# Attention scores of the three upper block levels, limited to the queries and keys that are read

## What is computed

```python
f = 1.0 / (1.0 + np.exp(-f_logit))
state = np.zeros((B, H, D, D), dtype=np.float32)
for t in range(S):
    state = f[:, :, t, :, None] * state + np.einsum('bhd,bhe->bhde', k[:, :, t], v[:, :, t])
    y[:, :, t] = np.einsum('bhd,bhde->bhe', q[:, :, t], state)
```

## Time and profile before

| | |
|---|---|
| median of 3 runs | 1319.17 us (1318.1 to 1324.99) |
| profiled execution, its own time | 1315.64 us |
| its span, first to last instruction | 1314.0 us |
| TensorE, matmuls | 1246.3 us busy, 95% |
| TensorE, stationary loads | 1148.2 us busy, 87% |
| VectorE | 859.2 us busy, 65% |
| ScalarE | 458.8 us busy, 35% |
| GpSimd | 454.3 us busy, 35% |

### The profile page before, as it was taken

One profiled execution on the slowest core, in us unless ns is written; L12 is line 12 of the kernel. 1 busy time (PEld: TensorE's weight loads), 2 busy tenths in 40 slices (PEclk: granted clock), 3 DMA queues, 4 the chain that ended last, 5 costly groups with the idle time before them and its releaser, 6 DMA issues.

```text
span 1314.0 us, 26515 instructions
## 1 busy us (share of the span) xinstructions
PE 1246.3 (95%) x8915; PEld 1148.2 (87%) x8916; DVE 859.2 (65%) x1939; ACT 458.8 (35%) x982; POOL 454.3 (35%) x376
## 2 busy tenths in 40 slices
PE   4899999999899999999999999599999999999998
PEld 3787887877798999989999898499999999999997
DVE  6888898885477878778787787344444544444433
ACT  3565566554222232222322222332332323233221
POOL 8558787654623506060536440310010101010000
PEclk9999999999999999999999999799999999999999
DMA  6233333253613131313313510210010101010000
GB/s 213 66 105 119 125 115 120 82 178 107 228 69 139 41 144 36 144 48 132 144 36 120 184 44 25 78 37 28 28 54 1 55 18 38 18 36 18 0 18 18
DMA packets 36175, 105.46 MB, mean 80 GB/s; under 512 B 4992, under 2 KB 20352, under 8 KB 33664
## 3 DMA queue, kind: packets, MB, share of 16 engines
q1 hardware_dynamic: 27504, 56.41, 13.0%
q0 software_dynamic: 8592, 47.98, 10.3%
HBM read 77.83 MB, written 26.54 MB: 79 GB/s over the span
## 4 chain that ended last, share of the span: by engine, by line
PE 76%; POOL 9%; DVE 7%; ACT 4%; issue 4%; DMA 1%; DVEq 0%; POOLq 0%; ACTq 0%
PE pD L1750 12%; PE pD L1859 10%; PE pA L1859 10%; PE pS L1782 8%; PE pA L1782 8%; PE pA L1873 7%; PE pA L1559 5%; PE pA L1750 4%; PE pS L1873 3%; PE pA L1764 2%; POOL fT L563 1%; PE pX L1724 1%; POOL prods L598 1%; DVE W L1070 1%; POOL we L688 1%
## 5 line engine op out<-in xcount | busy, mean ns | idle before, releaser
L1496 DVE TENSOR_TENSOR gs<-pD,sig 128x384 f32<-128x384 f32 x96 | 53.5, 557 | 199.6 <-ACT sig L1005 199.6
L1246 DVE STREAM_TRANSPOSE pA<-pD 32x128 f32<-32x128 f32 x416 | 138.3, 332 | 54.5 <-PE pD L1750 48.7
L739 POOL DMA_INDIRECT pair<-y_sorted,y_row x48 | 46.5, 969 | 340.7 <-DVE z L1475 271.7
L1246 DVE STREAM_TRANSPOSE pA<-pA 32x128 f32<-32x128 f32 x400 | 133.0, 332 | 44.0 <-PE pA L1750 38.4
L1559 PE MATMUL pA<-W 64*128 64x128 f32 x1920 | 141.6, 289 | 16.3 <-DVE W L1070 12.2
L909 ACT ACTIVATE hidH<-pA 128x512 fp32r<-128x512 f32 x110 | 65.5, 599 | 250.0 <-DVE pA L1246 246.4
L1559 PEld LDWEIGHTS pA<-W 64*128 64x128 f32 x1920 | 119.9, 192 | 34.8 <-DVE W L1070 18.7
L1750 PE MATMUL pD<-we,xsH 128*128 x462 | 146.0, 397 | 2.8 <-issue 2.8
L1782 PE MATMUL pA<-we,hidH 128*128 (+1 forms) x464 | 120.7, 341 | 0.0
L1005 ACT ACTIVATE sig<-pD 128x384 f32<-128x384 f32 x96 | 47.2, 491 | 210.4 <-PE pA L1859 210.4
L1070 DVE TENSOR_TENSOR W<-W,prods 128x512 f32<-128x512 f32 (+1 forms) x120 | 98.8, 829 | 28.9 <-PE pA L1559 26.8
(11 more groups left out here) (260 smaller groups left out, 2887.1 us busy)
## 6 DMA issues: line engine op xcount, KB each, us to landing
stage<-w POOLq DMA_DIRECT2D x14, 1536.0 KB, 8.9
qk<-qk_t SPq DMA_DIRECT2D x24, 512.0 KB, 3.7
xs<-x_sorted SPq DMA_DIRECT2D x55, 192.0 KB, 2.4
y_sorted<-yo SPq DMA_DIRECT2D x55, 192.0 KB, 1.9
fT<-f_t SPq DMA_DIRECT2D x12, 512.0 KB, 4.3
vN<-v_n SPq DMA_DIRECT2D x24, 256.0 KB, 2.7
out<-fin SPq DMA_DIRECT2D x8, 576.0 KB, 2.8
stage<-w SPq DMA_DIRECT2D x2, 1536.0 KB, 9.5
```

The source lines that it names most:

```text
L739: pool.indirect_dma_start(out=pair[:, j, k], out_offset=None, in_=y_sorted[:, :], in_offset=bass.IndirectOffsetOnAxis(ap=y_row[:, t * TS + ...
L1246: ins = dve.transpose(by_32[1][32 * q:32 * (q + 1), :, i], by_32[0][32 * i:32 * (i + 1), :, q])
L1496: dve.tensor_tensor(gs[:], pD[:, f % 2 * 512:f % 2 * 512 + TT], sig[f % 2][:], ALU.mult).then_inc(s_u, 1)
```

## The change

From level 3 on, `scores` hands the matmul fewer columns: of the keys (stationary) those up to the end of the last first half, 128 - h, and of the queries (moving) only the second halves', 64 of 128. The output shrinks in the same way: 128 - h partitions, and in each group of 128 columns only the second halves' columns, which are written where they were before. Level 3 has h = 16 (112 keys, queries in runs of 16), level 4 h = 32 (96 keys, runs of 32), level 5 h = 64 (64 keys, one run of 64). The number of matmuls, their order, all waits and all other engines' instructions stay as they are.

```diff
+def later_halves(v, h):
+
+    return v.rearrange("p (b s u) -> p b s u", s=2, u=h)[:, :, 1]
...
                 for c in range(HP):
                     for s in range(2):
                         r = slice(HS * s, HS * (s + 1))
-                        ins = pe.matmul(pA[par][:, s, c * P:(c + 1) * P], both[r, 1, c], both[r, 0, c],
-                                        start=True, stop=True)
+                        to, keys, queries = pA[par][:, s, c * P:(c + 1) * P], both[r, 1, c], both[r, 0, c]
+                        if n > MASKED - 1:
+                            h = LEVELS[n - 1]
+                            to, keys = later_halves(to[0:P - h], h), keys[:, 0:P - h]
+                            queries = later_halves(queries, h)
+                        ins = pe.matmul(to, keys, queries, start=True, stop=True)
```

## The result

**Measured: 1327.82 us** (median of 15 runs, 1323.87 to 1331.86) against 1320.22 us before (15 runs, 1315.64 to 1324.99). The ratio is 1.0064, 95% interval 1.0052 to 1.0077. The change makes the kernel slower by a little over the 0.5% that can be told from no change. Forecast were 1315.7 us and a range of 1309 to 1321: the prediction was wrong, in size and in sign. It had given "slower" 0.07.

The account below looks back on a forecast made before the run. TensorE and VectorE, both nearly full, wait for each other, with b5 on the loop setting the period. Gains of 1.95 + 0.96 + 0.64 = 3.5 us took 1319.17 to 1315.7 us, range 1309 to 1321.

Parts of the forecast that it names:

- What bounds the kernel: Attention pairs: TensorE and VectorE both nearly full and waiting for each other; of six changed sets only b5 sets the period.
- What one set saves: Scores: stationary columns set the step; levels 3, 4, 5 save 0.11, 0.21, 0.42 us, at most 17.8 us in all.
- The transitions: From each pair to the next: what of the saving reaches the end, mostly b5's 0.42 us, limited by later waits.
- Pairs 3, 6 and 9 at nothing: From b5 to the next a1 after a sequence's end: a1 starts right behind VectorE's first mask, so 0 us gained.
- Pairs 5 and 8: From b5 to the next a1: a1 can start sooner only until VectorE's first mask limits it, 0.23 us each.
- The 0.96 us from pair 0 to pair 1: At half clock b5 ends over 1 us sooner, removing VectorE's wait for it: 0.96 us gained, no more.
- 0.64 on levels 3 and 4: Pair 11, up to the end of b4: the saving reaches VectorE and what follows attention, 0.64 us gained.
- rival 4: TensorE does less, so its clock falls more often, each 3.4 us costing up to 1.7: 1317 to 1322 us; chance 0.05.
- Rival 1: Pairs: shorter a3 to a5 pull VectorE forward, 0.6 us a pair or more, down to 1301 us; chance 0.16.
- Rival 2: Changed sets: the step follows neither operand, so nothing is saved, 1319 to 1320 us; chance 0.12.
- Rival 3: Levels 3 and 4: writing output in runs slows the matmuls, 30 us in all, 1349 us; chance 0.05.
- The additional change of shape: Level 5's 64 by 64 shape: 0.1 us at a5, hidden in a wait, so nothing; not hidden, 1.2 us.

Follow-up runs that it names:

- e15: The change plus five unused matmuls a pair in TensorE's waits (pairs 1 to 11) and the first expert's weights fetched a pair earlier: 1314.96 us, ratio 0.9991 to before.
- e13: Kernel before with level 5 alone cut and the first expert's weights fetched a pair earlier: 1313.29 us, ratio 0.9981 to before.
- e2: The change with only the keys (stationary) cut in levels 3 to 5, queries whole: 1319.94 us, ratio 0.9995 to before.
- e1: The change with only the queries (moving) cut in levels 3 to 5, keys whole: 1351.87 us, ratio 1.0219 to before.
- e8: The kernel before, unchanged, run once for a second trace: 1314.38 us.
- e14: The kernel before with only the first expert's weights fetched a pair earlier: 1316.66 us, ratio 1.0003 to before.
- e12: The change, unaltered, run once for a second trace: 1331.39 us.
- e9: The change plus five unused matmuls a pair in pairs 1 to 11, three before b4 and two before a5: 1319.05 us, ratio 0.9994 to before.
- e6: Kernel before with level 5 alone cut, in both tiles, levels 3 and 4 whole: 1313.57 us, ratio 0.9992 to before.
- e4: The change with both sets of level 5 computed twice into the same place: 1340.34 us, ratio 1.0160 to before.
- e11: The kernel before plus eight unused matmuls behind pair 11: 1317.58 us, ratio 0.9993 to before.
- e5: Kernel before with levels 3 and 4 cut as in the change, level 5 whole: 1322.63 us, ratio 1.0058 to before.

## Why the prediction was wrong

**What bounds the kernel: right.** TensorE was busy for 94% of the span, and 15.8 us less in the changed sets gave nothing. Waits for W took up most of what a3 to a5 saved: the view of waits grew by 9.4 us, and e15, which cuts levels 3 and 4 as well and fills the waits, has no period more than 0.16 us shorter than e13's. In pairs 3, 6 and 9 a5 did count, which comes below. No run cuts levels 3 and 4 without either falls or fills.

**What one set saves: right in size, from a wrong reason.** Level 3 spans 0.743 us from first to last start (0.78 expected), level 4 0.650 (0.68) and level 5 0.463 (0.47), before 0.890. I had written that the stationary side sets the step and that moving columns come free below it. e2 with 64 stationary and 128 moving columns spans 0.821 us and refutes the first half: in these runs mainly the larger operand sets it. The change cuts both, so the number held. The rule of the Trainium skill that stood against the row (TensorE: Matmul & The Clock Gate, part 2, "Step-by-step", phase 3: throughput is purely the moving columns) isn't what these runs show: by it e1's sets would be 0.44 us shorter, and they are 0.05 us shorter.

**The transitions: a sum that was right, with terms that weren't.** Pairs 3, 6 and 9 at nothing was wrong, nearly 0.5 us each, since I looked at what a1 waits for and not at whether b5 itself waited. Pairs 5 and 8 gave 0.12 and 0.14 of the 0.23. The 0.96 us from pair 0 to pair 1 hung on a fall of the clock that isn't in every execution: b5 of pair 1 starts at 60.84 in the first trace and at 59.09 in e8, the same kernel. In pair 11 I named no late transfer; it took 0.93 us back. That e13 starts its last b5 3.5 us ahead of e14, the sum to a tenth, is luck: of the 3.5 predicted, 0.96 hung on a fall that neither of the two has and 0.64 on levels 3 and 4, which e13 leaves whole. In their place stand above all the 1.4 us of pairs 3, 6 and 9.

**The step that failed: the sum has no term for the clock.** It put the clock's part at nothing, and that part was 9.2 us, more than twice the sum and of the other sign. The reason for the nothing is rival 4, "The clock falls more often because TensorE does less", with "later pairs have shorter waits. Some 1317 to 1322 us" and a chance of 0.05. The mechanism was named and then priced from what I could see at one place, the fall at 36.8 us. Three things were wrong in it. It was argued from waits, and e1 has shown a falling clock with half the moving columns and no longer waits (10.1 us against 10.3 in e2 and 9.8 in e8). It was counted as a few falls, and there are nine (in e12 eight). And it was taken as apart from the forecast, though the forecast's own saving, short sets with waits behind them in every pair, is what brings it on. The price for each was in order: the falls cost 1.0064 less 0.9994, 9.2 us, for 34 to 38 us at half clock more than in e9, so 0.8 to 0.9 us for each 3.4, within the "up to 1.7". With nine falls of which three last 6.8 us, my own figure (41.0 less 3.4 us of them, 1.7 for each 3.4: 18.8) would have given some 1334 at the most. e1 is nearer to it: its last b5 is 34 us behind e8's, for 82 us at half clock up to there, 1.4 for each 3.4.

**The other rivals.** Rival 1 (more comes through): no pair shortened by 0.6 us; the nearest is 0.49. Rival 2 (no saving): refuted by the three spans. Rival 3 (runs in the output): refuted by the same spans and by e1; the Trainium skill (PSUM — Partial Sum Buffer, "Specifications (TRN2)") warns of access patterns that aren't contiguous, and runs of 16 and 32 fp32 columns cost nothing that can be seen here, with a stationary side that is larger than the 64 moving columns. The additional change of shape is not visible in any ratio (e6, 0.9992, has the 64 by 64 sets in full).

## What to carry to other kernels

Where TensorE and another engine wait for each other, take work out of TensorE only where a set lies on the loop: here level 5 gave all of the gain there was and levels 3 and 4 nearly all of the loss. Before pricing a cut in matmul work by its duration, look in the trace for any place at which the granted clock falls, see what TensorE did before it, and ask where the change makes more such places; test it by filling the new waits with matmuls that nobody reads. And when a phase gets shorter, look up which transfers at its end are issued behind something else in the queue, for they will be the next to be late.

## What the runs showed of the hardware that I had not expected

- **Fewer moving columns can cost clock with TensorE as busy.** e1 and e2: a share of 0.936 in both outside the falls, but a clock of 0.86 against 1.00, and 1.0219 against 0.9995.
- **A useless matmul can save time**: e9 against the change, 0.9994 against 1.0064.
- **A set of fp32 matmuls, two heads side by side, needs both operands cut** to get shorter: 0.837 us with one side at 64, 0.821 with the other, 0.463 with both, 0.890 with neither.
- **The column of the granted clock can miss a stretch.** In e4 it says 1.00 where the matmuls take twice their time, and TensorE in order of time shows it (a0 of pair 7 in two rows, 1.89 us from its first to its last start instead of 0.89; logit_parts 1.36 us instead of 0.64):

```profile
183.58 1.36 PE L1642 MATMUL pD<-yT,wr 128*32 128x256 f32 x8
184.87 1.42 PE L1569 MATMUL pA<-qk 64*128 64x128 f32 x11
186.53 0.51 PE L1569 MATMUL pA<-qk 64*128 64x128 f32 x5 [0.24 <-issue]
```

```profile
182.60:189.50 6.90, 6.12 (x79) 4.31 (x80) 2.86 (x6) 2.28 (x5) 3.18 (x4) 1.00 0.32 118
```

  That a fall went unrecorded is inferred from the durations. The duration of a set that is known at full clock is the surer sign.
- **A stall of ScalarE of some 3 us, put down to "remote"**, between two activations (hidH) of the second expert tile. Two rows, one of the change and one of e11:

```profile
333.15 0.60 ACT L914 ACTIVATE hidH<-pA 128x512 fp32r<-128x512 f32 x1 [2.95 <-remote]
```

```profile
325.12 0.60 ACT L909 ACTIVATE hidH<-pA 128x512 fp32r<-128x512 f32 x1 [3.01 <-remote]
```

  e11 has the attention of the kernel before. On the two chips of e1 to e4 and of e9 to e12 every trace has this stall, 2.66 to 3.11 us, with or without the change (in e9 it is put down to "issue"); on the chip of e5 to e8 and e13 to e15 none has it. So in these runs it goes with the chip, and its cause wasn't tried. Of the first two traces, whose chip isn't on record, only the change's has it. Whoever reads the 10.0 us between the two profiled spans as the change's would count 3 of them wrongly; the medians say 7.6 in all.
